# A second token block's first layer as seven half-size products, with the weights' sums made by GpSimd during the first two blocks

## The reference: what is computed

```python
state = gamma * state + outer(k[t], v[t]);  y[t] = scale * q[t] @ state   # attention, 4 x 8 heads
h = x @ w_in                       # 3072 x 512 by 512 x 2048
g = where(h >= 1, h, where(h <= -1, 0, (h + 1)**2 / 4))
x2 = g @ w_out                     # 2048 x 512
# then: h2 = x2 @ w2_in, softmax gate, layer norm, @ w2_out
```

## Time and profile before

| | us |
|---|---|
| median of 3 runs | 854.63 (854.13 to 855.33) |
| the profiled execution's own time | 854.29 |
| its span in the profile | 852.4 |
| TensorE busy | 845.9, 99% of the span |
| VectorE, ScalarE, GpSimd busy | 538.1, 351.9, 266.1 |

### The profile page before, as it was taken

The page is one execution under the profiler, slowest core; times in us unless marked ns, Lnnn a source line. Parts: engine busy times, 40 slices in busy tenths (PEclk is TensorE's granted clock), DMA queues, the critical chain, the costliest instruction groups (busy, mean ns, idle before and its releaser), DMA issues.

```text
span 852.4 us, 13606 instructions
## 1 busy us (share of the span) xinstructions
PE 845.9 (99%) x5248; PEld 714.4 (84%) x5248; DVE 538.1 (63%) x985; ACT 351.9 (41%) x546; POOL 266.1 (31%) x242
## 2 busy tenths in 40 slices
PE   8999999999999999999999999999999999999998
PEld 7788888888988888888988888888887888888886
DVE  5545557665655476545854563567888898898831
ACT  3333443223422243222522232256466766675642
POOL 2654632325323342233412113236441112221000
PEclk9999999999999999999999999999999999999999
DMA  9921207565344444444353414200166554455351
GB/s 339 376 74 64 67 28 253 201 223 170 123 132 153 125 132 144 147 144 130 109 175 112 123 40 148 99 26 25 42 212 177 163 173 148 149 185 169 128 171 64
DMA packets 70976, 120.71 MB, mean 142 GB/s; under 512 B 7040, under 2 KB 25472, under 8 KB 70912
## 3 DMA queue, kind: packets, MB, share of 16 engines
q1 hardware_dynamic: 70336, 119.32, 42.9%
q10 hardware_dynamic: 576, 0.52, 0.2%
HBM read 86.26 MB, written 33.55 MB: 141 GB/s over the span
## 4 chain that ended last, share of the span: by engine, by line
PE 94%; DMA 2%; DVE 1%; SPq 1%; issue 1%; POOL 0%; ACT 0%; DVEq 0%
PE acc L637 31%; PE h L607 15%; PE o_ps L1433 14%; PE h L539 14%; PE p L1333 11%; PE att L482 3%; PE att L493 2%; PE att L517 1%; PE att L507 1%; DMA z<-zq 1%; DMA q<-in_q 1%; DMA x_raw<-x2T 1%; PE acc L493 0%; PE h L624 0%; SPq L315 0%
## 5 line engine op out<-in xcount | busy, mean ns | idle before, releaser
L637 PE MATMUL acc<-g_hi,w 128*128 128x512 f32 x768 | 258.4, 398 | 0.0
L1129 POOL TENSOR_TENSOR g_lo<-g_raw,g_hi 128x512 fp32r<-128x512 f32 x96 | 132.6, 1382 | 351.3 <-ACT g_hi L681 351.3
L637 PEld LDWEIGHTS acc<-g_hi,w 128*128 128x128 f32 x768 | 144.3, 188 | 35.4 <-issue 3.4
L758 ACT ACTIVATE g_raw<-g_raw,half_bias 128x512 f32<-128x512 f32 x96 | 69.2, 721 | 234.8 <-DVE g_raw L984 234.8
L637 PE MATMUL acc<-g_lo,w 128*128 128x512 f32 x384 | 150.1, 391 | 0.0
L607 PE MATMUL h<-x_hi,w 128*128 128x512 f32 x376 | 123.7, 390 | 0.0
L997 DVE TENSOR_TENSOR h<-h 128x256 f32<-128x256 f32 x144 | 60.9, 423 | 93.7 <-PE h L539 65.8
L984 DVE TENSOR_SCALAR g_raw<-h 128x512 f32<-128x512 f32 x96 | 54.1, 563 | 77.0 <-PE acc L637 75.7
L681 ACT ACTIVATE g_hi<-g_raw 128x512 fp32r<-128x512 f32 x96 | 60.7, 632 | 83.9 <-DVE g_raw L989 83.9
L989 DVE TENSOR_TENSOR g_raw<-h,g_raw 128x512 f32<-128x512 f32 x96 | 66.8, 696 | 36.7 <-ACT g_raw L758 36.6
L637 PEld LDWEIGHTS acc<-g_lo,w 128*128 128x128 f32 x384 | 72.2, 188 | 13.1
(11 more groups left out here) (141 smaller groups left out, 1448.6 us busy)
## 6 DMA issues: line engine op xcount, KB each, us to landing
s<-w_sums SPq DMA_DIRECT2D x96, 256.0 KB, 2.7
z<-zq SPq DMA_DIRECT2D x24, 512.0 KB, 2.8
zt<-z SPq DMA_DIRECT2D x92, 128.0 KB, 3.0
kT<-in_kT SPq DMA_DIRECT2D x24, 256.0 KB, 3.5
q<-in_q SPq DMA_DIRECT2D x24, 256.0 KB, 2.9
v<-in_v SPq DMA_DIRECT2D x24, 256.0 KB, 3.5
x2T<-y SPq DMA_DIRECT2D x24, 256.0 KB, 2.6
x_raw<-x2T SPq DMA_DIRECT2D x12, 512.0 KB, 4.6
```

The lines of the kernel that those rows point to most:

```text
L637: last = mm(acc[m][:, :], ww, gg[:, f % 2, :], start=f == 0 and t == 0, stop=f == FT1 - 1 and t == 2)
L758: nc.scalar.activation(gate[:, f % 2, :], gate[:, f % 2, :], ACT.Square, bias=half_bias[:, 0:1], scale=0.5).then_inc(sem["squared"], 1)
L1129: tt(g[1][:, f % 2, :], gate[:, f % 2, :], g[0][:, f % 2, :].bitcast(F32), ALU.subtract)\
```

## The change

Block 1 becomes a seven-product block too (`SEVEN` is blocks 1 to 4). So the sums of weights have to exist earlier. GpSimd makes them: those of pairs 0, 1 and 2 in block 0, at steps 6, 8 and 10 (`PREPARE_AT`), those of pairs 3 to 7 in block 1, each three pairs ahead of its use (`AHEAD`). ScalarE's `sums_high` in block 0 stands one step later, VectorE's `sums_low` two steps later; in block 1 all three stand in the same pair. Pairs 0 and 2 are made in `s`, the others in a buffer of its own, `s_made`, over which lies `x_sum`. The splits of a plain `x` (`split_y`) go. SyncE's queue is rewritten: transfers of pairs and sums stand between the attention's loads of block 1's chunks, and ahead of `load_sum` in block 1.

```diff
-SUMS_BLOCK = 1
-SEVEN = range(SUMS_BLOCK + 1, BLOCKS - 1)
+SEVEN = range(1, BLOCKS - 1)
-PREPARE_AT = (0, 1, 3, 4, 6, 7, 9, 10)
+PREPARE_AT = (6, 8, 10)
+AHEAD = len(PREPARE_AT)
+def stage_of(i):
+    return 0 if i in (0, 2) else 1
...
# SyncE, ahead of block 1
-            for c in range(B + 1, 2 * B + 1):
-                load_kT(c)
-                load_rest(c)
             load_pair(0)
+            load_kT(B + 1)
+            load_rest(B + 1)
+            load_kT(B + 2)
             load_pair(1)
-            store_x2(0)
...
+            load_rest(B + 2)
+            store_sums(0)
+            load_pair(2)
+            load_kT(B + 3)
+            load_rest(B + 3)
+            store_sums(1)
+            load_pair(3)
+            load_kT(2 * B)
+            store_sums(2)
+            load_rest(2 * B)
# SyncE, in the loop over pairs
+                    if blk == SEVEN[0] and 1 <= p <= FPAIRS - AHEAD:
+                        if p < FPAIRS - AHEAD:
+                            load_pair(p + AHEAD)
+                        store_sums(p + AHEAD - 1)
# ScalarE, dense and pair
+                        if f - 1 in PREPARE_AT:
+                            sums_high(PREPARE_AT.index(f - 1))
-                    if blk == SUMS_BLOCK and f in PREPARE_AT:
-                        sums_high(PREPARE_AT.index(f))
+                if q + AHEAD < FPAIRS:
+                    sums_high(q + AHEAD)
                 square(blk, f)
# VectorE, pair and dense
+                if q + AHEAD < FPAIRS:
+                    sums_low(q + AHEAD)
-                    if blk == SUMS_BLOCK:
-                        if f - 1 in PREPARE_AT:
-                            sums_low(PREPARE_AT.index(f - 1))
-                        if f in PREPARE_AT:
-                            sums_of_weights(PREPARE_AT.index(f))
+                    if blk == 0 and f - 2 in PREPARE_AT:
+                        sums_low(PREPARE_AT.index(f - 2))
# GpSimd
+            def sums_of_weights(i):
+                raw, out = mem["w_pair"], mem["s_raw"][stage_of(i)]
+                low_k, high_k = slice(0, HALF), slice(HALF, BLK)
+                pool.wait_ge(sem["pair_loaded"], 16 * (i + 1))
+                if i == 2:
+                    pool.wait_ge(sem["s_stored"][0], 16)
+                elif i > 2:
+                    pool.wait_ge(sem["s_stored"][1], 16 * (i - 2))
+                    pool.wait_ge(sem["x_lo"], x_parts(SEVEN[0]))
+                tt(out[:, 2, 1, :], raw[:, 1, low_k], raw[:, 1, high_k], ALU.add).then_inc(sem["s_summed"], 1)
+                tt(out[:, 0, 1, :], raw[:, 0, low_k], raw[:, 1, low_k], ALU.subtract).then_inc(sem["s_summed"], 1)
+                pool.wait_ge(sem["s_summed"], 4 * i + 1)
+                tt(out[:, 1, 1, :], out[:, 2, 1, :], raw[:, 0, low_k], ALU.subtract).then_inc(sem["s_summed"], 1)
+                pool.wait_ge(sem["s_summed"], 4 * i + 3)
+                tt(out[:, 3, 1, :], raw[:, 0, high_k], out[:, 1, 1, :], ALU.subtract).then_inc(sem["s_summed"], 1)
                 attention(blk + 1, 4 * p)
                 attention(blk + 1, 4 * p + 1)
+                if q + AHEAD < FPAIRS:
+                    sums_of_weights(q + AHEAD)
...
                         for piece in w_out_at(f):
                             split_weights(piece)
+                        if f in PREPARE_AT:
+                            sums_of_weights(PREPARE_AT.index(f))
```

More of the change, by code:

```diff
@@ L182, in place @@
     plain("state", [P, B, PAIRS, D])
-    x3_at = cursor[0]
     split("x3", [P, 3, 2, HALF])
-    plain("x_sum", [P, 3, 2, HALF])
     s_at = cursor[0]
     mem["s"] = [put("s", [P, 4, 2, HALF], F32R)]
+    sums_at = cursor[0]
+    mem["s"].append(put("s_made", [P, 4, 2, HALF], F32R))
+    mem["x_sum"] = put("x_sum", [P, 3, 2, HALF], F32, at=sums_at)
+    plain("w_pair", [P, 2, 512])
     plain("h", [P, 2, BLK])
-    mem["w_pair"] = put("w_pair", [P, 2, 512], F32, at=cursor[0] - 8 * BLK)
     end = cursor[0]
     assert end <= nc.sbuf_usable_end, (end, nc.sbuf_usable_end)
-    mem["s"].append(put("s_x3", [P, 4, 2, HALF], F32R, at=x3_at))
-    mem["s_raw"] = [put(f"s_raw{n}", [P, 4, 2, HALF], F32, at=at) for n, at in enumerate((s_at, x3_at))]
+    mem["s_raw"] = [put(f"s_raw{n}", [P, 4, 2, HALF], F32, at=at) for n, at in enumerate((s_at, sums_at))]
     cursor[0] = w_at + FIRST_PIECE * 8192
@@ L708, in split_part @@
                 copy(x_part(name, 0), x_raw(name)).then_inc(sem["x_hi"], 1)
-            def split_y(blk, kt):
-                act.wait_ge(sem["y_done"], blk * B)
-                act.wait_ge(sem["h_ready"], blk * FT1)
-                copy(x[0][:, kt, :], y[:, kt, :]).then_inc(sem["x_hi"], 1)
             def copy_first(q):
@@ L769, in dense @@
                 for f in range(steps(blk)):
-                    if f == FT1 - 1 and blk + 1 < SEVEN[0]:
-                        for kt in range(KT):
-                            split_y(blk + 1, kt)
                     if f == FT1 - 2 and blk + 1 == SEVEN[0]:
@@ L902, in split_part @@
                     .then_inc(sem["x_lo"], 1)
[L904 to L920 removed]
             def sums_low(i):
+                n = stage_of(i)
                 dve.wait_ge(sem["s_hi"], i + 1)
[L924 removed]
+                tt(s[n][:, :, 1, :], mem["s_raw"][n][:, :, 1, :], s[n][:, :, 0, :].bitcast(F32),
                    ALU.subtract).then_inc(sem["s_lo"], 1)
@@ L1791 @@
         "warm w_in_hi w_out_hi w0_in_lo w_in_lo w_out_lo "
-        "pair_loaded s_summed s_hi s_lo products1 part1 taken1 x_summed x_hi x_lo h_ready clamped squared gmax g_hi g_lo g_used "
+        "pair_loaded s_summed s_hi s_lo products1 part1 taken1 x_summed x_hi x_lo "
+        "h_ready clamped squared gmax g_hi g_lo g_used "
         "w2_summed w2_in_hi w2_in_lo w2_out_hi w2_out_lo x2_summed x2_hi x2_lo products part_copied taken "
```

49 lines of the change are left out of this document (11 added, 38 removed).

## The result

| | before | after |
|---|---|---|
| median, us | 854.39 (853.91 to 855.33, 13 runs) | 856.58 (856.02 to 857.67, 13 runs) |
| ratio | | 1.0026, 95% interval 1.0018 to 1.0034 |
| profiled execution, its span | 854.29, 852.4 | 856.61, 854.8 |

What follows compares the result with a forecast made beforehand. TensorE, busy 99% of the span at full clock, was taken as the bound. The terms -3.15 + 3.8 + 0.2 gave +0.85 us: 855.5 us on the median of 854.63, likeliest case 853.9 to 857.1, 8 in 10 within 852.3 to 858.0.

Steps and rivals of the forecast that it cites:

- likeliest case: Whole kernel: about no change, end of block 0 costing 2.5 to 4.8 us, block 1's pairs up to 1; chance 0.45.
- Term 1: TensorE in block 1: one plain block becomes a seven-product block, 3.15 us less.
- Term 2: End of block 0: added work delays `down(13)`, P1 and P2 through GpSimd and VectorE, 3.8 us more.
- lower bound of 1.1: End of block 0: with sums costing nothing, `w_out` splits still make P2 1.1 us late.
- step 11: Block 0: `sums_high(2)` waits for GpSimd's sums of pair 2 until 94.3; `clamp(12)` starts 1.35 us late.
- step 10: Block 0: until here added work only eats slack, `low(f)` ending some 4 to 7 us ahead of `down(f)`.
- Term 3: Pairs of block 1: two circles of waits add 0.2 us, from 0 to about 3.
- circle through ScalarE: Block 1, pairs 0 to 4: clamp to sums to `sums_high` to next clamp, 11.2 to 13.7 us a pair.
- the second one, through DRAM: Block 1: next sums wait in `s_made` for the store, 4.7 us to land, within 0.3 us of GpSimd's asking.
- rival 2: Block 1: the circle decides, pairs 1 to 4 each later, `down` of even steps waiting; 858.3 us; 0.29 with Rival 3.
- Rival 1: End of block 0: sums hide, saving stays, sums of x by 104.5; -2.05 us, 852.6 us; chance 0.26.
- Rival 3: Block 1: TensorE does not save 3.15 us, as late transfers could add 5 us; 0.29 with rival 2.

Runs made afterwards that it cites:

- e4: Changed kernel without GpSimd's sums of weights of pairs 0, 1 and 2, ScalarE copying plain quarters of `w_in` instead; 856.20 us, ratio 1.0022 to before.
- e6: Changed kernel with e1, e3, x's parts reordered, `low(13)` between the sums of x, GpSimd's last `w_out` split a step later; 853.53 us, ratio 0.9988 to before.
- e1: Changed kernel with GpSimd's sums of pair 1 behind the key scaling of step 9 in block 0, not ahead; 855.90 us, ratio 1.0014 to before.
- e3: Changed kernel with VectorE's mask of the next block's scores ahead of `larger` in pairs 0 to 4 of block 1; 856.04 us, ratio 1.0022 to before.
- e9: Changed kernel with sums of pair 1 behind the key scaling and ScalarE's square and high ahead of `sums_high`; 855.41 us, ratio 1.0013 to before.
- e8: Kernel of e6 with ScalarE's square and high ahead of `sums_high` in every pair; 852.95 us, ratio 0.9983 to before.
- e10: Changed kernel with GpSimd's `low(13)` between the second and third of the four sums of x; 860.41 us, ratio 1.0069 to before.
- e2: Changed kernel with t4's split last of the seven at the end of block 0, not ahead of `clamp(14)`; 855.60 us, ratio 1.0015 to before.
- e5: Changed kernel with VectorE's `sums_low` of block 0 one step later each (steps 9, 11, 13); 857.91 us, ratio 1.0037 to before.

## Why the prediction was right in its range and short in its size

The measured 856.58 lies in the likeliest case's own range, 853.9 to 857.1. But the prediction also put "no change" at 1.7 us either way, and 2.2 us (1.5 to 2.9) is over that line, though not with its whole interval. The mechanism of the likeliest case came true and its size was short; by the split of the chances the result falls, narrowly, to "slower", which had 0.29 and for which I had named other causes.

**Term 1** (3.15 us less) held. Block 1 is busy 98.59 us where the plain one took 101.63, and blocks 2 and 3 cost 98.47 and 98.49.

**Term 2** (the end of block 0, +3.8) held to the tenth: 3.76. I had put `down(13)` 2.0 late and it is 115.33 - 112.20 - 1.15 = 1.98 late; P1 2.65 and it is 2.59 (3.74 less the 1.15 at the update). That agreement has luck in it, since several steps were each some tenths off: GpSimd's sums of x began at 107.40, which less the unforeseen 1.15 is 106.25 and not 106.7. e4 shows what was behind term 2: with GpSimd's sums left out, it is 3.57. So GpSimd's own sums of weights are only 0.2 of it. What is left is the work of GpSimd and VectorE taking turns: `sums_low`, the splits of `w_out`, and then the four sums of x ahead of `low(13)`. How the 3.57 divides among these is read from the timelines and not shown by a run, since none leaves `sums_low` out; nor is my lower bound of 1.1 tested, which left it out too. That the order in which x's parts are made and split lets TensorE feel it is shown: with the order of e6 P1 is not late at all. My step 11, in which GpSimd's sums of pair 2 delay `sums_high(2)`, was right as a chain (their end at 95.3, ScalarE late behind them) but worth only the remaining 0.2.

**The step that failed** is the sentence that "until step 10 the added work only eats slack". I looked at `low` and `down` there, not at the key scaling, whose consumer is the attention's update on TensorE. GpSimd's sums of pair 1 end at 80.1 and push the scaling to 81.1; TensorE wanted it at 80.2. That is 1.15 us, the larger half of what was missing (e1).

**Term 3** (+0.2, from 0 to 3) was too small: 0.6, in pair 4 alone (e3, e9). The circle through ScalarE that I named is real: square behind `sums_high` behind GpSimd's sums. So is the second one, through DRAM: I had the store land within 0.3 us of when GpSimd asks, and by the times in e3 GpSimd waits for it 0.94 us in pair 2 and 1.59 in pair 4. What gives way in it is the mask behind `larger`, whereas I expected `down` of an even step; rival 2's growing stall from pair to pair did not come.

So the sum should have read -3.15 + 1.15 + 3.76 + 0.6 = 2.36. Against the 0.85 forecast, the 1.15 and 0.4 of term 3 were missing. Rival 1 did not come about: it needed the sums of x at 104.5, and even e4 has them at 106.1. Rival 3 neither: none of TensorE's five gaps in these blocks is ended by a transfer, though the store just named stands in the chain behind the last of them.

**The port.** The pair sums cost 0.73 to 0.75 us each (I took 0.72), 0.92 to 1.00 in three cases in block 1, and 1.71 and 1.72 where a `sums_low` was beside them; `sums_low` took 2.31 there instead of 1.22. So the four sums of pair 1 and of pair 2 took 3.9 us and not 3.0. Whole operations took turns, as the earlier trace rows had it, and where I carried these turns forward the numbers came out.

What stays open: of e8's remaining 1.0 us in block 1 the gaps explain most, not each tenth; and e1 and e9 show executions 1.7 and 2.3 us apart (854.6 to 856.9). A clock drop in some executions and not in others explains at most a part: the two slowest of e9 have its lowest mean clocks, 0.995 and 0.997, but the three fastest of e1 have 0.997 and 0.998, and one of 856.31 has 1.000.

## What to carry over

- When work is added to an engine's queue, list every consumer of what stands behind it, on every engine, in each step up to the first wait; the one I left out was an engine with no slack at all. Slack in the gate chain says nothing of slack in the attention.
- An operation that will wait (here a rounding for sums that come late) should stand behind, not ahead of, whatever is ready and on the way to TensorE: moving ScalarE's square ahead of it was worth 1.2 us of D in e8.
- A gap on TensorE need not be a cost by itself. Removing the one at `down(13)` alone made the kernel slower (e10); the order in which the next block's inputs are prepared was what had to change. Together, the changes of order turned a loss of 2.2 us into a gain of 1.5.

## What the runs showed of the hardware

TensorE's granted clock falls to half behind short gaps, and not every time. Behind the same gap of 1.83 us ahead of `down(13)` it stayed at 1.00 in the profiled executions of the changed kernel, e2, e3 and e9, and went to 0.50 (1.2 GHz) for about 3 us in e1, 1.4 us after TensorE had gone on. In e5 (2.55 us) and e10 (3.43 us) it fell to 0.50 while TensorE still waited; in e10 it stayed there for over 6 us, which cost 1.8 us on top of the gap. All four executions of e10 show a mean clock of 0.994 to 0.996, against 0.998 to 1.000 in those of the changed kernel. Where TensorE would have waited anyway, as in e1, the slower clock cost nothing measurable.
